# Two stages in one block: GpSimd mixes the first half during the last attention pair, and four w_k units stand in the drain

## The reference

```
scores = q @ k^T / sqrt(64)
attn   = exp(scores - max) where scores >= max - tau, else 0;  rows divided by their sum
x      = (attn @ v), heads side by side                      # (8, 576, 512)

xk = mu_k * x + (1 - mu_k) * x_prev                          # x_prev: x one position earlier
xr = mu_r * x + (1 - mu_r) * x_prev
x2 = sigmoid(xr @ w_r) * (relu(xk @ w_k)^2 @ w_v)

gate = sigmoid(causal convolution of x2 over 5 positions)
out  = (gate * (x2 @ w_val)) @ w_out
```

## Time and profile before

| | |
|---|---|
| median of 3 runs | 1322.56 us (1321.21 to 1323.99) |
| the profiled execution | 1316.92 us, its span 1315.1 us |
| TensorE busy | 1282.8 us (98%) |
| DVE, ScalarE, GpSimd busy | 891.0, 839.9, 334.5 us |
| mean granted clock of TensorE | 0.991 |

### The profile page before, as it was taken

How to read it: one execution, slowest core, us unless ns; L and a number is a source line. 1 busy time by engine, 2 the same in 40 slices (tenths; PEclk the granted TensorE clock), 3 DMA queues, 4 the chain that set the end, 5 groups by cost and what they waited for, 6 DMA issues and landing times.

```text
span 1315.1 us, 29612 instructions
## 1 busy us (share of the span) xinstructions
PE 1282.8 (98%) x9396; PEld 1136.1 (86%) x9396; DVE 891.0 (68%) x1969; ACT 839.9 (64%) x2023; POOL 334.5 (25%) x385
## 2 busy tenths in 40 slices
PE   7999999999999999969999999999999999999998
PEld 7777777777777777749999999999989999999997
DVE  4777777777777777757666665657655766566644
ACT  4888888888888888855544453455445544544432
POOL 2466665666666654421000000000000000000000
PEclk8999999999999999989999999999999999999999
DMA  6455566565655555421001101110110011001000
GB/s 148 114 150 154 152 162 164 155 158 157 153 151 148 153 147 148 113 79 45 9 27 36 35 9 37 35 35 1 35 44 23 15 35 35 16 27 35 17 9 32
DMA packets 137821, 105.19 MB, mean 80 GB/s; under 512 B 92416, under 2 KB 109056, under 8 KB 137728
## 3 DMA queue, kind: packets, MB, share of 16 engines
q1 hardware_dynamic: 136224, 103.41, 29.1%
q10 hardware_dynamic: 1504, 0.62, 0.2%
HBM read 54.56 MB, written 19.02 MB: 56 GB/s over the span
## 4 chain that ended last, share of the span: by engine, by line
PE 54%; DVE 1%; ACT 0%; issue 0%; DVEq 0%
PE kv_ps L897 16%; PE kv_ps L978 15%; PE vr_ps L897 15%; PE y_ps L962 8%; DVE mixed L1090 0%; DVE xm_lo L1096 0%; ACT mixed L1010 0%; DVE x L1149 0%; ACT xm_hi L1018 0%; ACT y L1027 0%; DVE x_lo L1154 0%; DVE square L1107 0%; DVE g_lo L1122 0%; DVE gated L1117 0%; ACT x_hi L1074 0%
## 5 line engine op out<-in xcount | busy, mean ns | idle before, releaser
L654 DVE TENSOR_REDUCE neg_max<-score_ps 128x1 f32<-128x576 f32 x288 | 212.6, 754 | 71.5 <-PE score_ps L506 71.2
L659 DVE SCALAR_TENSOR_TENSOR probs<-score_ps,threshold,probs 128x576 f32<-128x576 f32 x288 | 228.0, 808 | 45.0 <-ACT probs L589 44.0
L589 ACT ACTIVATE probs<-score_ps,neg_max 128x576 f32<-128x576 f32 x288 | 212.8, 739 | 0.0
L506 PE MATMUL score_ps<-k_lo,q_all 128*128 128x288 f32 x640 | 193.7, 332 | 7.5 <-DVE probs L659 5.3
L571 ACT ACTIVATE probsT<-aux_ps 128x512 f32<-128x512 f32 x288 | 164.6, 598 | 36.2 <-PE aux_ps L467 32.0
L467 PE MATMUL aux_ps<-ident,probs 128*128 128x128 f32 x1280 | 186.0, 276 | 0.1
L506 PE MATMUL score_ps<-k_hi,q_all 128*128 128x288 f32 x640 | 172.6, 297 | 0.0
L467 PEld LDWEIGHTS aux_ps<-ident,probs 128*128 128x128 f32 x1280 | 148.9, 142 | 18.7 <-ACT probsT L571 15.2
L897 PE MATMUL kv_ps<-xm_hi,w_lo 128*128 128x288 f32 x512 | 152.3, 298 | 12.3 <-DVE xm_lo L1096 9.5
L897 PE MATMUL kv_ps<-xm_hi,w_hi 128*128 128x288 f32 x512 | 152.2, 297 | 0.0
L897 PE MATMUL kv_ps<-xm_lo,w_hi 128*128 128x288 f32 x512 | 152.1, 297 | 0.0
(11 more groups left out here) (93 smaller groups left out, 2959.6 us busy)
## 6 DMA issues: line engine op xcount, KB each, us to landing
q_all<-q_lo SPq DMA_DIRECT2D x62, 160.0 KB, 3.3
recip_rows<-recip_scratch SPq DMA_DIRECT2D x64, 144.0 KB, 3.1
x_scratch<-x_out SPq DMA_DIRECT2D x32, 288.0 KB, 2.2
out<-y SPq DMA_DIRECT2D x36, 256.0 KB, 2.0
v_nat<-in_v SPq DMA_DIRECT2D x32, 256.0 KB, 3.1
qk_nat<-in_q SPq DMA_DIRECT2D x63, 128.0 KB, 2.6
qk_nat<-in_k SPq DMA_DIRECT2D x63, 128.0 KB, 2.6
k_hi<-k_hi SPq DMA_DIRECT2D x32, 160.0 KB, 2.7
```

The source lines that it names most:

```text
L506: last = nc.tensor.matmul(ps[:, half, 0:HALF], query(h, i, par), kk[:, par, at:at + HALF], start=(n == 0), stop=(n == len(terms) - 1))
L589: nc.scalar.activation(tile_halves(i), scored(i), ACT.Exp, bias=neg_max[:, i:i + 1], scale=1.0).then_inc(exp_done, 1)
L654: nc.vector.tensor_reduce(neg_max[:, i:i + 1], scored(i), mybir.AxisListType.XY, ALU.max, negate=True).then_inc(max_ready, 1)
L659: nc.vector.scalar_tensor_tensor(tile_halves(i), scored(i), threshold[:, i:i + 1], tile_halves(i), ALU.is_ge, ALU.mult, accum_out=row_sum[ ...
```

## The change

Both stages stand in one block, so the barrier between them is gone. The two stages' tensors in SBUF share addresses, their PSUM banks become the same (w_k and w_v products use `score_ps` 0 and 1, w_r and w_val products `score_ps` 2, those with w_out `aux_ps`), and the orders below keep them apart.

- GpSimd mixes half 0 (`mixed_ahead`): part 0, for w_k, between `sums` and `normalize` of pair 30, while pair 31 is scored; part 1, for w_r, between `sums` and `normalize` of pair 31. Each is 20 instructions of 288 columns. ScalarE and DVE no longer mix half 0.
- `x_first` is loaded right after the store of pair 29, before SyncE's steps of pair 31, and GpSimd's `sums` of pair 30 waits for it.
- TensorE's last steps are written out (`PE_DRAIN`): four units of w_k products stand between them, and `rem1` comes later. The mixing stage then starts with unit 4.
- SyncE loads the x of half 1 before w_out, where w_out came first, and after it has waited for the store of pair 31.
- q_all, k_hi and k_lo are two tensors each instead of one with two parts.

```diff
+PE_DRAIN = steps("""
+    probs5- pv0- probs6- probs4- hidden0 probs7- probs8- hidden1 rem1- hidden2 pv1- hidden3
+""")
+ACT_DRAIN = steps("probs3- probs5- exp8- pv0- probs6- probs4- probs7- probs8- rem1- pv1-")
+DVE_DRAIN = steps("max8- mask8- recip0-")
...
                 run(0, PAIRS - 2)
-                run(0, PAIRS - 1)
                 sp.dma_start(*x_first).then_inc(small_loaded, 16)
+            run(0, PAIRS - 1)
                 run(0, PAIRS)
                 sp.wait_ge(x_moved, 16 * (PAIRS + 1))
-                sp.wait_ge(small_loaded, 16 * (len(small_loads) + 1))
...
-                for c in range(PAIRS - 1, PAIRS + 1):
-                    run(0, c)
+            wait(small_loaded, 16 * (len(small_loads) + 1))
+            wait(q_stacked[1], count_loaded(0, PAIRS - 1, 2))
+            sums(0, PAIRS - 2)
+            mixed_ahead(pool, 0)
+            normalize(0, PAIRS - 2)
+            sums(0, PAIRS - 1)
+
+            wait(aux_copied, turns(0, number_of(PAIRS - 1, "rem", 0) + 1))
+            mixed_ahead(pool, 1)
+            normalize(0, PAIRS - 1)
...
+                    elif kind == "hidden":
+
+                        pe.wait_ge(probs_ready, count(it, PAIRS - 1, TILES, MASK_TURN[6 + i // 2] + 1))
+                        pe.wait_ge(w_split, 2 * UNITS + 2)
+                        hidden_ahead(pe, i)
...
+        def mixed_ahead(pool, i):
+
+
+            if i == 0:
+                nc.gpsimd.memset(x_in[:, :, 0:1], 0.0).then_inc(x_edge, 1)
+                nc.gpsimd.tensor_scalar(one_mu[:], mu[:], -1.0, 1.0, ALU.mult, ALU.add).then_inc(one_mu_ready, 1)
+                pool.wait_ge(one_mu_ready, 1)
+                pool.wait_ge(x_edge, 1)
+            else:
+                pool.wait_ge(mix_lo_ready, C)
+            for n in range(C):
+                nc.gpsimd.tensor_scalar(mixed[:, n, :], x_in[:, n, 0:HT], one_mu[:, i, n:n + 1], None,
+                                        ALU.mult).then_inc(mix_prev, 1)
+
+            own = (relu, y)[i]
+            for n in range(C + 1):
+                if n < C:
+                    if n >= 2:
+                        pool.wait_ge(mix_done, C * i + n - 1)
+                    nc.gpsimd.tensor_scalar(own[:, n % 2, 0:HT], x_in[:, n, 1:HT + 1], mu[:, i, n:n + 1], None,
+                                            ALU.mult).then_inc(mix_own, 1)
+                if n > 0:
+                    pool.wait_ge(mix_prev, C * i + n)
+                    pool.wait_ge(mix_own, C * i + n)
+                    nc.gpsimd.tensor_tensor(mixed[:, n - 1, :], own[:, (n - 1) % 2, 0:HT], mixed[:, n - 1, :],
+                                            ALU.add).then_inc(mix_done, 1)
+            for n in range(C):
+                pool.wait_ge(mix_done, C * i + n + 1)
+                nc.gpsimd.tensor_copy(xm_hi[i][:, n, :], mixed[:, n, :]).then_inc(mix_hi_ready, 1)
+            for n in range(C):
+                pool.wait_ge(mix_hi_ready, C * i + n + 1)
+                nc.gpsimd.tensor_tensor(xm_lo[i][:, n, :], mixed[:, n, :], xm_hi[i][:, n, :].bitcast(F32),
+                                        ALU.subtract).then_inc(mix_lo_ready, 1)
...
                         sp.wait_ge(mix_done, count(it, c, 2 * C, 2 * C))
                         load_x(it, c + 1)
+                if first:
+                    load_w_out()
```

More of the change, by code:

```diff
@@ L1 @@
+from collections import namedtuple
 from contextlib import ExitStack
@@ L684, in turn @@
+        return Engines(sync, gpsimd, tensor, scalar, vector)
 def turn(text):
@@ L889, in _, with run @@
-            @block.tensor
-            def _(pe):
-                def split_products(ps, terms, before_term=lambda i: None):
+            def run(it, c, first, last):
+                if not last and not (c == N - 1):
+                    sp.wait_ge(mix_done, count(it, c, 2 * C, 2 * C))
+                    load_x(it, c + 1)
+                if first:
+                    load_w_out()
+                if not first:
+                    store_y(it, c - 1)
+            halves(run, sp)
+            for i in range(2):
+                sp.wait_ge(y_moved[i], 16 * C // 2 + 16 * y_count(0, N, i))
@@ new lines, in split_products, with mixes, wait @@
+        def split_products(ps, terms, before_term=lambda i: None):
+            n = 0
+            for i, (wh, wl, mh, ml) in enumerate(terms):
+                before_term(i)
+                for w, m in ((wl, mh), (wh, mh), (wh, ml)):
+                    last = nc.tensor.matmul(ps, w, m, start=(n == 0), stop=(n == 3 * len(terms) - 1))
+                    n += 1
+            return last
+        def mixes(pe, it, c, j, which):
+            def wait(n):
+                if j == 0:
+                    pe.wait_ge(mix_lo_ready, count(it, c, 2 * C, C * which + n + 1))
+            return wait
@@ L1193, in thresholded_attention_then_mixing, with _ @@
         x_first = (x_in[:, :, 1:HT + 1], x_scratch[0:C, :, 0:HT].rearrange("c p t -> p c t"))
-        attention(nc, q, k, v, tau, small, x_first, sources, x_scratch, recip_scratch, w_hi, w_lo)
-        mixing(nc, x_scratch, mu, taps, x_in, w_out, out, w_hi, w_lo, *starts)
+        mix, mixed_ahead, hidden_ahead = mixing(nc, banks, semaphore, x_scratch, mu, one_mu, taps, x_in, w_out, out,
+                                                w_hi, w_lo, *starts)
+        att = attention(nc, banks, semaphore, q, k, v, tau, small, x_first, sources, x_scratch, recip_scratch,
+                        w_hi, w_lo, mixed_ahead, hidden_ahead)
+        with nc.Block() as block:
+            @block.sync
+            def _(sp):
+                att.sync(sp)
+                mix.sync(sp)
+            @block.gpsimd
+            def _(pool):
+                att.gpsimd(pool)
+                mix.gpsimd(pool)
+            @block.tensor
+            def _(pe):
+                att.tensor(pe)
+                mix.tensor(pe)
+            @block.scalar
+            def _(act):
+                att.scalar(act)
+                mix.scalar(act)
+            @block.vector
+            def _(dve):
+                att.vector(dve)
+                mix.vector(dve)
 _INS = ["q", "k", "v", "tau", "moe_mu_k", "moe_mu_r", "moe_w_k", "moe_w_v", "moe_w_r",
```

1279 lines of the change are left out of this document (628 added, 651 removed).

## The result

| | before | after | ratio, 95% interval |
|---|---|---|---|
| beside each other | 1321.62 us (7 runs, 1319.44 to 1323.99) | 1315.46 us (7 runs, 1312.7 to 1320.26) | 0.9956 [0.9936, 0.9975] |
| once more, later | 1318.76 us (17 runs) | 1316.08 us (12 runs, 1310.21 to 1320.21) | 0.9977 [0.9966, 0.9989] |

The change makes the kernel faster, by 6 us in one measurement and 3 in the other, where I had forecast 11.35.

What follows compares the result with a forecast made beforehand. TensorE, busy 98% of the span, was taken as the bound, so only its waits and slow clock at the seam counted. 14.9 - 1.9 - 0.45 - 1.2 = 11.35 us off 1322.56 gave 1311.2, range 1308.5 to 1316.5.

Steps and rivals of the forecast that it cites:

- T: GpSimd's mixing of one half: 8 TENSOR_SCALAR, 8 TENSOR_TENSOR, 4 CAST and waits; 12.4 us, 10.7 and 15.2 at the bounds.
- the sum: Seam between the stages: 14.9 us gained, less 1.9 for late x, 0.45 for w_out splits, 1.2 for the clock: 11.35.
- The rival's own formula: "Slower than before", GpSimd's queue: x of half 1 lands at 567.55 + 2T; 1325.3 us at T = 20; chance 0.04.
- row_sum near 556.8: GpSimd's row_sum of pair 30 waits for half 0's x, which lands 4.0 us after issue; 0.5 us late.
- 12 to 13 us per half: Sign on GpSimd: each half's mixing takes 12 to 13 us, with TENSOR_SCALAR near 0.46.
- No idle in front of the x_raw copy: Sign on ScalarE: its x_raw copy for the last pair, behind GpSimd's normalize of pair 30, is not held up.
- The cover of 1.1: Slack of 1.1 us between normalize of pair 30 and ScalarE's x_raw copy; past it, every us goes onto the drain.
- Unit 4 near 584.2: TensorE starts w_k unit 4 there instead of at 599.10, clock 1.0 until then; 14.9 us gained.
- x for half 1 near 594.0: SyncE's load lands then, behind the second mixing, normalize and pair 31's store; ScalarE waits some 2 us; minus 1.9.
- A wait of 2.8 us for r_tanh, then half clock: TensorE idles from 593.7 to 596.5, then runs at half clock; the clock's price minus 1.2 us (0 to 1.9).
- w_v 49.0 after the store: First w_v product near 601.4 instead of 612.76, with the same distance from there to the end.
- the drain's fillers: w_k units in TensorE's drain fill the 0.78 us wait for probsT; part of the 14.9 us gained.

Runs made afterwards that it cites:

- cheap_form: The changed kernel with GpSimd's sixteen TENSOR_SCALAR products as TENSOR_TENSOR against a broadcast column; 1306.38 us, 0.9912 of the kernel before.
- second profile: The changed kernel profiled again later with no edit, the fastest of its twelve runs; 1310.21 us.
- first profile: The changed kernel's first profiled execution, the slowest of its seven runs; 1320.26 us.
- half1_early: The changed kernel with half 1's x loaded once half 0 is mixed, ahead of the store of pair 31; 1310.01 us, 0.9926 of the kernel before.
- both_behind: Both early x loads on the changed kernel, but the old drain order with all w_k units behind it; 1307.23 us, 0.9922 of the kernel before.
- block_alone: The changed kernel without GpSimd's mixing and without w_k units in the drain; one block and new load order stay; 1313.69 us, 0.9951 of before.
- both_cheap: Both early x loads plus the TENSOR_TENSOR form of GpSimd's sixteen products, on the changed kernel; 1302.01 us, 0.9871 of the kernel before.
- part1_act_dve: The changed kernel with both early x loads, and part 1 of the mixing on ScalarE and DVE within the drain; 1307.72 us, 0.9914 of before.
- units_behind: The changed kernel with the old drain order, all eight w_k units in the mixing stage; 1316.05 us, 0.9966 of the kernel before.
- both_early: The changed kernel with half 0's x loaded one pair earlier and half 1's ahead of pair 31's store; 1307.75 us, later 1306.70; 0.9916 and 0.991.
- first_early: The changed kernel with half 0's x loaded one pair earlier and GpSimd's sums ahead of its wait; 1312.85 us, 0.995 of the kernel before.

## Why the prediction was right in direction and too large

**The term that was mis-sized** is T, the mixing of one half on GpSimd. The prediction had "TENSOR_SCALAR with a per-partition scalar is not shown at width. It has one streamed input, like CAST; I take 0.46, with bounds of 0.25 [...] and 0.81". It takes 1.0. Eight of them add 4.3 us to T; the casts give back 0.3 and the 0.5 for waits isn't seen, so 15.9, where 15.65 is measured. cheap_form changes only this price (T = 12.81), and its seam gains 60.38 - 49.23 = 11.15 us against the 11.35 of the sum. The mechanism was right, and this price took most of what was missing. The rival's own formula, x_in landing at 567.55 + 2T, shows it too: with the 15.68 and 16.58 us of the second profile it gives 599.8, or 47.4 us after the store of pair 29, and ScalarE took x_in 48.1 after it. A smaller miss is the landing of the first load.

That cheap_form meets the sum within 0.2 us is in part luck: its unit 4 was 1.0 us late and its wait for r_tanh 0.45 longer than forecast, and the 1.2 us for the clock didn't come.

**Point by point**, in the order of the prediction's list:

1. *row_sum near 556.8*, 4.4 us after the store of pair 29: 4.6 in the second profile, 6.1 in the first. The 4.0 us to land are the median of the eight loads of half 1's kind; this load took 5.2 to 5.5 in five of the seven profiles in which it stands behind that store. In the four of them in which GpSimd's `sums` waits for it, TensorE waits 1.8 to 2.2 us for a mask where I charged 0.35, with a fall of the clock behind it that the sum doesn't have (0.50 for 566 to 568 in the first profile). GpSimd's whole chain starts 1.5 us later then; the two seams are 2.8 apart.
2. *12 to 13 us per half*: 15.65 and 17.46. Part 1 was longer than part 0 by more than the 0.4 that I gave it, since four casts took 2.45 instead of 1.54 and four subtracts 3.96 instead of 3.06, beside DVE's squares (in the second profile, 15.68 and 16.58, the subtracts alone).
3. *No idle in front of the x_raw copy*: ScalarE waited 1.31 and 2.82 us, TensorE 0.60 and 2.11. The cover of 1.1 was about right: part 0 is 3.3 longer, and 2.1 of that comes through in the second profile.
4. *Unit 4 near 584.2, 31.8 us after the store*: 36.1 in the second profile (unit 3 at 585.43 and 1.58 on), where the clock also fell to 0.61 for 574 to 578; 32.8 with cheap_form, at full clock.
5. *x for half 1 near 594.0, 41.6 after the store*: ScalarE took it 48.1 and 50.1 after. The path was as described; both parts' excess counts in it.
6. *A wait of 2.8 us for r_tanh, then half clock*: 4.67 and 6.83, with the clock at 0.50 behind both. Its price there was 1.8 us: the 24 products up to w_v took 5.13 us, in cheap_form 3.36. cheap_form waited 3.25 us and saw no fall; half1_early's clock fell after 2.34. So my 1.2 is a cost that comes in some executions and not in others, and not one that the length of the wait decides.
7. *w_v 49.0 after the store*: 55.7 and 58.5; 49.2 with cheap_form. From there to the end 701.4 us, before 702.3: the rest was unchanged, as said.

**What the sum had right by luck.** It credits the drain's fillers (0.78 for pv1) and the absence of the barrier together with 14.9. both_behind shows that the units' place is worth nothing measurable there, and block_alone that one block with the new order of loads brings as much as the change did. The start of 599.10 from which the sum counts also held what half 0's mixing on DVE was stretched beside GpSimd's w_out splits (12.7 us, 7.9 in block_alone), and no term names that. A gain of that size is nevertheless there: both_cheap's seam gains 14.7, once nothing waits for x.

**What stays open.** The two measurements of the same change differ (0.9956 and 0.9977, intervals that just overlap), more than the profiled seams explain: those gain 1.9 and 4.7 us, the medians 6.2 and 2.7. Why the load for half 0 lands later right behind the store of pair 29 than one pair earlier, and not in every execution, isn't known. How part1_act_dve would do with w_out split later wasn't tried.

## What to carry to other kernels

An instruction form that the trace doesn't show at width has no upper bound from a "similar" one: here the form with fewer streamed operands was the slower, and a short kernel that times it alone would have settled the forecast. When work is moved to an idle engine, count it in each chain that passes through that engine's queue: these parts stood in one chain twice, and 2.9 and 3.3 us too much in them (the second profile against cheap_form) went with 6.5 us between the seams, falls of the clock included. Try the smallest part of a change by itself, and move loads to the first point at which their buffer is free, not behind a store that they don't need.

## What the runs showed of the hardware

- GpSimd, 288 columns of float32 in SBUF: TENSOR_SCALAR 1.00 us (0.93 with a constant), TENSOR_TENSOR 0.80, TENSOR_TENSOR against a broadcast column 0.67, CAST 0.385. The Trainium skill (GPSIMD Engine Reference, Engine selection) calls one-input work on GpSimd "roughly line-rate"; by that these would be near 0.49 (my estimate in the prediction). The CAST is under that, the TENSOR_SCALAR twice as long, and the measurement decides.
- DVE's squares, 0.45 us alone, took 0.67 beside GpSimd's casts, 1.06 beside its subtracts and 1.55 beside the 512-wide normalize, and GpSimd's own casts and subtracts stretched too (0.385 to 0.61, 0.77 to 0.99). This agrees with the rule of the Trainium skill on the shared ports (SBUF — State Buffer, SBUF: two separate sides). Where GpSimd was done sooner (both_cheap), fewer squares were stretched.
- The granted clock fell to 1.2 GHz (0.50) behind waits of TensorE of 4.67 us and more each time. Behind shorter ones it fell in some executions: after 1.78 us in units_behind, 1.96 in both_early's second profile, 2.02 in part1_act_dve, 2.34 in half1_early, 2.45 and 3.57 in block_alone. It did not fall after 1.96 in both_behind, 2.02 in first_early, 2.37 in both_early's first profile, 2.80 in part1_act_dve or 3.25 in cheap_form. Among waits of 1.8 to 3.3 us, none of these runs shows what decides.
- A load of 576 KB from HBM issued right behind the store of pair 29 landed after 5.2 to 5.5 us in five profiles and 4.0 and 4.5 in two; one pair earlier it took 4.0 to 4.4 in six.
